# Slot tables of a routed expert layer: splits and requests of the next expert's weights in larger groups

## The reference, cut to what matters

```python
e_idx = np.argmax(x @ w_gate, axis=1)          # x: 4608 tokens x 512
for e in range(8):
    mask = e_idx == e
    h = np.maximum(x[mask] @ w1[e], 0.0)       # w1[e]: 512 x 1024
    ye = h @ w2[e]                             # w2[e]: 1024 x 512
    out[mask] = gate_w[mask, None] * eom[mask, e, None] * ye
```

## Time and profile before

| what | value |
|---|---|
| runs, median (lowest to highest) | 1189.59 us (1189.06 to 1194.86), 3 runs |
| profiled execution, span from the first to the last instruction | 1192.1 us |
| mean granted TensorE clock | 0.975 |
| TensorE matmul busy | 1120.0 us, 94% |
| VectorE, ScalarE, GpSimd busy | 612.4, 422.1, 204.2 us |
| share of TensorE in the chain that ended last | 92% |
| routed stage | from the first `S_ps`, 671.7 us, to the last `Y`, about 1181 us |

### The profile page before, as it was taken

One profiled execution on the slowest core, in us unless ns is written; L12 is line 12 of the kernel. 1 busy time (PEld: TensorE's weight loads), 2 busy tenths in 40 slices (PEclk: granted clock), 3 DMA queues, 4 the chain that ended last, 5 costly groups with the idle time before them and its releaser, 6 DMA issues.

```text
span 1192.1 us, 23624 instructions
## 1 busy us (share of the span) xinstructions
PE 1120.0 (94%) x6468; PEld 929.2 (78%) x6469; DVE 612.4 (51%) x1285; ACT 422.1 (35%) x788; POOL 204.2 (17%) x375
## 2 busy tenths in 40 slices
PE   3799999999999999999998399999999999999795
PEld 2688888888888888888886388888888888888584
DVE  6666666767577666767673443432424342342410
ACT  4244334443444344433442033433333342332320
POOL 2244021202111121102101211111111111111110
PEclk9899999999999999999998599999999999999898
DMA  8542222222221222122200234432333333133000
GB/s 216 124 125 84 59 72 70 53 53 71 70 57 49 70 71 68 43 66 71 53 10 27 81 116 119 144 117 91 113 106 115 107 104 107 60 106 97 28 28 26
DMA packets 155831, 96.73 MB, mean 81 GB/s; under 512 B 127630, under 2 KB 127758, under 8 KB 155792
## 3 DMA queue, kind: packets, MB, share of 16 engines
q1 hardware_dynamic: 145728, 75.61, 22.3%
q0 software_dynamic: 7968, 20.61, 5.8%
q10 hardware_dynamic: 2096, 0.04, 0.1%
HBM read 76.66 MB, written 20.60 MB: 82 GB/s over the span
## 4 chain that ended last, share of the span: by engine, by line
PE 92%; DVE 2%; DMA 2%; issue 1%; ACT 1%; SPq 1%; POOL 0%; ACTq 0%; DVEq 0%; POOLq 0%
PE Y_ps L416 35%; PE H_ps L416 35%; PE T L408 9%; PE S_ps L483 3%; PE X_ps L463 3%; PE X_ps L408 3%; PE L_ps L438 2%; PE S_ps L408 1%; DVE wx L676 1%; DMA stage<-in_moe_w_out 1%; DMA stage<-in_k 0%; SPq L298 0%; SPq L308 0%; DMA prob<-x_rows,slot_rec 0%; ACT wx L570 0%
## 5 line engine op out<-in xcount | busy, mean ns | idle before, releaser
L416 PE MATMUL Y_ps<-wx,dh 128*128 (+1 forms) x1216 | 386.9, 399 | 2.1 <-DVE dl L676 2.0
L416 PE MATMUL H_ps<-wx,xh 128*128 (+1 forms) x1216 | 338.3, 401 | 10.8 <-DVE wx L676 8.7
L416 PEld LDWEIGHTS H_ps<-wx,xh 128*128 128x128 f32 x1216 | 226.5, 191 | 55.6 <-issue 12.0
L416 PEld LDWEIGHTS Y_ps<-wx,dh 128*128 128x128 f32 x1216 | 221.0, 189 | 43.5 <-issue 2.4
L416 PE MATMUL Y_ps<-wx,dl 128*128 (+1 forms) x608 | 238.3, 392 | 0.0
L416 PE MATMUL H_ps<-wx,xl 128*128 (+1 forms) x608 | 189.4, 393 | 0.0
L676 DVE TENSOR_TENSOR wx<-stage,wx (+1 forms) x62 | 75.4, 1224 | 158.5 <-ACT wx L632 156.6
L416 PEld LDWEIGHTS H_ps<-wx,xl 128*128 128x128 f32 x608 | 115.7, 190 | 24.8
L416 PEld LDWEIGHTS Y_ps<-wx,dl 128*128 128x128 f32 x608 | 114.5, 188 | 25.4
L766 DVE COPY x2T<-T 128x512 f32<-128x512 f32 x36 | 24.9, 691 | 121.2 <-PE T L408 112.0
L976 POOL TENSOR_TENSOR var<-sumsq,rden 128x1 f32<-128x1 f32 x36 | 6.8, 188 | 462.8 <-ACT stage L609 462.8
(11 more groups left out here) (164 smaller groups left out, 1399.3 us busy)
## 6 DMA issues: line engine op xcount, KB each, us to landing
stage<-in_moe_w SPq DMA_DIRECT2D x128, 256.0 KB, 3.0
stage<-in_q SPq DMA_DIRECT2D x72, 128.0 KB, 2.8
stage<-in_k SPq DMA_DIRECT2D x72, 128.0 KB, 3.2
stage<-in_v SPq DMA_DIRECT2D x72, 128.0 KB, 3.1
x_rows<-x SPq DMA_DIRECT2D x36, 256.0 KB, 2.9
stage<-in_moe_w_in SPq DMA_DIRECT2D x6, 256.0 KB, 3.8
stage<-in_moe_w_out SPq DMA_DIRECT2D x6, 256.0 KB, 4.5
slot_rec<-route_table SPq DMA_DIRECT2D x40, 2.0 KB, 1.6
```

The lines of the kernel that those rows point to most:

```text
L416: i = pe.matmul(acc[:, c0:c0 + HALF], x[:, kk, :], w(part, kk * cols + c0), start=first and x is hi and part == 0, stop=last and x is lo)
```

## The change

Two constants become three. They enter only the tables.

```diff
-SPLIT_RATE = 2
-LOAD_RATE = 2
+SPLIT_RATE = 5
+SPLIT_FIRST = 3
+LOAD_RATE = 4
...
             link(dve.tensor_scalar(idx, idx, float(SPLIT_RATE), None, ALU.mult))
             dve.tensor_scalar(mid, idx, float(PIECES), float(PIECES), ALU.min, ALU.add)
-            link(dve.tensor_scalar(idx, idx, 1.0, float(PIECES), ALU.add, ALU.min))
+            link(dve.tensor_scalar(idx, idx, float(SPLIT_FIRST), float(PIECES), ALU.add, ALU.min))
```

## The result

The changed kernel takes 1290.62 us in the median (1289.59 to 1292.74, 4 runs), the kernel before 1192.22 us beside it (1189.06 to 1195.55, 4 runs). The ratio is 1.083, with a 95% interval of 1.080 to 1.086: slower by about 98 us.

The account below looks back on a forecast made before the run. It took the routed stage to be bound by back-to-back TensorE slots. Experts 1 to 5 +71, expert 0 +33, expert 7 -3.4, another `Y` wait +0.9: +101 us, so 1290 us in the median, range 1260 to 1318.

Parts of the forecast that it names:

- The mechanism: Experts 1 to 5: the third record follows five SyncE steps, 47.9 us after `H` of local slot 1 starts.
- The wait per expert: Experts 1 to 5, local slot 4: TensorE's `S_ps` waits once for gathered rows, 10.2 us.
- The clock: TensorE behind each of seven long waits: runs slower, costing 2.2 us each time.
- Faster* rival: Wait ahead of expert 7 falls by two fifths, nothing replaces it, clock kept: 1184 to 1186 us; chance 0.02.
- Expert 0: First expert: `S_ps` waits of 10.5, 1.9 and 14.2 us; with `Y` and clock 33 us in all.
- no wait of its own: Expert 0, local slot 1: the last early-requested piece reaches ScalarE's end loop late but adds no separate wait, 0 us.
- The end loops of three: Local slots 0 and 1: the second `dl` ends later, delaying `Y` 0.9 us each time, 2.0 in expert 0.
- Expert 7: First slot of expert 7: expert 6 leaves three pieces instead of six, so the `H` wait falls 8.7 to 5.3 us.
- The signs of being wrong: Burst steps under 4.5 us, TensorE not waiting for an expert's third record, or ScalarE awaiting raw pieces after expert 0.
- the shorter steps: SyncE's queue: steps following one another take only 4.7 us, giving about 1265 us; chance 0.07.

Follow-up runs that it names:

- 3, 4, 1 run: The change with SyncE's steps limited to 3, 4, 1 per local slot in place of the split count: 1270.30 us, ratio 1.0640 to the kernel before.

## Why the prediction was right, point by point

- **The mechanism.** TensorE waits for a gather that waits for a record that stands behind five serial steps in SyncE's queue. Shown by the rows of after, and by two runs that take it away from either side: spread steps (no long waits in experts 1 to 5), and records in another queue (none at all). The third record of the second expert is issued at 824.94; `H` of its local slot 1 began at 778.63, so this is T+46.3, where 47.9 was worked out. In the other experts it is T+45.8 to T+48.9.
- **The wait per expert**, 10.2 us worked out, 9.1 measured (8.67, 10.66, 7.60, 9.51, 8.97). Two terms were a little too large: the second to fourth steps of the bursts of five take 4.8 to 5.2 us, 4.96 in the mean of 18, not 5.1, and the gather lands after 3.4 us in the median, not 3.9; the late one has no piece on its way beside it. One was too small: the first step of these bursts, with a gather and a store beside it, takes 5.6 to 6.5 us, 5.9 in the mean, not 5.7.
- **The clock**, 2.2 us per long wait, measured 2.3 in the mean (the seven stretches are 9.77, 8.44, 9.14, 9.29, 8.50, 8.78 and 8.89 us, against 6.69). An eighth stands beside them that the sum took at nothing: behind the wait of 2.54 us in slot 3 the granted clock was 0.81 and the stretch 8.91 us, 1.7 us over what its own `Y_ps` wait explains. Together 17.7 us, where 15.4 were in the sum. In the slot behind the `H_ps` wait the clock's cost fell only from 2.2 to 1.6 us (13.86 us at 0.88), so a wait of 5.28 us was not short enough to keep the clock, which the *Faster* rival needed.
- **Busy time** is 22.0 us up, and not all of it is the clock. The last matrix products ahead of a wait have nothing behind them to overlap with, so their full length counts as busy: an ordinary `S_ps` is given 0.60 us, and `Y` starts 0.35 us after it. That is some 0.25 us at each `Y_ps` wait and 0.16 at each `S_ps` wait, 4.5 us in all. It has to be added to the idle time if one asks what a wait costs.
- **Expert 0**, `S_ps` waits of 10.5, 1.9 and 14.2 us worked out, 9.98, 2.54 and 11.04 measured. The third is shorter because TensorE came later and not because the rows came earlier: they landed at 757.9, where 758.0 was worked out, but TensorE, slowed behind the 2.54 us, wanted them at 746.9 instead of 743.8. The sentence that the late raw pieces have "no wait of its own" was right in the change and only there: it is 9.4 us once the other is gone.
- **The end loops of three**, 0.9 us each: the idle time is 0.5 to 0.7, but the slots are 0.7 to 1.0 us longer than 12.24, 0.86 in the mean of eleven, and slot 1 of expert 0 is 1.9 us longer, where 2.0 was worked out. A twelfth, in slot 3, was not in the sum; its idle time is 0.28 us.
- **Expert 7**, 8.7 to 5.3 us, measured 5.28.
- **The signs of being wrong** did not come: no step of the bursts is under 4.5 us, the third record is the one waited for, and ScalarE waits for raw pieces five times, all in expert 0, the last time at 710.62.

The sum in the trace: 69.0 (`S_ps`) + 6.8 + 1.7 (`Y_ps`) - 3.4 (`H_ps`) + 22.0 (busy time) = 96.1 against 95.7 of the spans. Put in the prediction's terms, with the lost overlap added to the waits, it is 70.3 (`S_ps`) + 11.9 (`Y_ps`) - 3.4 (`H_ps`) + 17.7 - 0.6 (clock) = 95.9. The forecast had 77.6 + 11.9 - 3.4 + 15.4 = 101.5. So the one term that was clearly mis-sized is that of the `S_ps` waits, too large by 7.3 us; the clock was too small by 1.7. That 1290 was hit to within a microsecond is luck. The sum was 6 us too large; against that, the median of before beside these runs was 1192.2, 2.6 us higher than the one that the sum was laid on, and the medians lie 98.4 us apart where the profiled executions lie 95.7.

Of the rivals, the shorter steps were nearest: the steps behind the first did turn out shorter than taken, but by 0.1 us in the mean, the first ones were longer, and the time is far from 1265. By the Trainium skill's rule ("DMA: Bandwidth & Descriptors", Anatomy of one DMA), which is stated for GpSimd's path, the estimate for a step was 4.7 us; the measured 4.96 in the mean without a gather beside it is 0.3 over that, and 5.9 with one is not near it.

## What to carry to other kernels

A queue that issues both bulk requests and small messages on which the next work depends makes the message wait for the bulk. When each bulk request also waits for the one before it to land, the price is (number of requests) x (round trip), and what decides is the room of the message, not the bandwidth: here 6 us of room, 5 us a request, and DMA engines busy for a quarter of the time (0.25 from 697 us to the end). So before a planner's rates are raised, count the steps between two messages and their round trips; or give the messages another queue, which took back 83 of the 98 us here. And look under a removed wait: two waits that end together hide one another. When a stretch is measured, take both of its ends from the trace, and when a wait is priced, take how much longer its slot is and not its idle time alone: here that was 0.9 us against 0.6.

## What the runs showed of the hardware

- A weight piece of two 256 KB parts took 4.8 to 5.2 us from request to next request in the middle of the bursts of five, and 5.6 to 6.5 in their first step, with a gather and a store beside it. A gather took 3.2 to 3.7 us from its start to its late use with no piece beside it (the change), and 4.3 to 5.0 with one (the 3, 4, 1 run).
- After TensorE stood still for 7.6 to 11.0 us, the granted clock was 0.69 to 0.81 over the 8.4 to 9.8 us that followed, so a part of them at 1.2 GHz and the rest at 2.4 GHz, at a cost of 1.7 to 3.1 us each time. After the wait of 5.78 us in the 3, 4, 1 run it was 0.75 over 8.88 us, at a cost of 2.2 us.
